# Gated attention in front of a soft mixture of experts and a tanh block: heads scored apart in 64x64 tiles, blocks of 64 tokens, one VectorE product a level

## The reference

```python
# q, k, v, f_logit: batch 4, heads 8, tokens 768, head_dim 48
f = 1.0 / (1.0 + np.exp(-f_logit))
state = zeros(B, H, D, D)
for t in range(S):
    state = f[:, :, t, :, None] * state + einsum('bhd,bhe->bhde', k[:, :, t], v[:, :, t])
    y[:, :, t] = einsum('bhd,bhde->bhe', q[:, :, t], state)
x = y as (3072 tokens, 384)
x = soft mixture of experts (x; phi 384x32, w1 8x384x1024, w2 8x1024x384)
out = (h - tanh(h)) @ w_out,  h = x @ w_in            # 384 -> 2048 -> 384
```

## Time and profile before

| what | value |
|---|---|
| time, median of 3 runs | 676.52 us (674.4 to 677.11) |
| span of the profiled execution, its own time | 674.4 us |
| PE busy | 581.7 us, 86%, 4505 instructions |
| DVE busy | 542.1 us, 80%, 970 |
| ACT busy | 214.4 us, 32%, 462 |
| POOL busy | 231.9 us, 34%, 294 |
| DMA | 55.39 MB, mean 82 GB/s |

### The profile page before, as it was taken

One profiled execution on the slowest core, in us unless ns is written; L12 is line 12 of the kernel. 1 busy time (PEld: TensorE's weight loads), 2 busy tenths in 40 slices (PEclk: granted clock), 3 DMA queues, 4 the chain that ended last, 5 costly groups with the idle time before them and its releaser, 6 DMA issues.

```text
span 674.4 us, 14283 instructions
## 1 busy us (share of the span) xinstructions
PE 581.7 (86%) x4505; PEld 504.7 (75%) x4505; DVE 542.1 (80%) x970; ACT 214.4 (32%) x462; POOL 231.9 (34%) x294
## 2 busy tenths in 40 slices
PE   4888878888888878888878888679999999999997
PEld 3767767677767767677765733269999999999997
DVE  4999999999999999999994642497777777777773
ACT  1233332334333332334323550312323223232322
POOL 3566565665666565665652000560000000000000
PEclk9899999999999999999999798879999999999999
DMA  5324433335253260533600689600100001010101
GB/s 102 69 44 91 127 70 111 70 60 156 41 139 70 52 163 17 146 76 63 205 1 1 201 287 394 242 0 1 48 0 16 31 0 47 0 47 0 47 1 47
DMA packets 118405, 55.39 MB, mean 82 GB/s; under 512 B 101616, under 2 KB 114928, under 8 KB 118000
## 3 DMA queue, kind: packets, MB, share of 16 engines
q1 hardware_dynamic: 118384, 55.11, 29.8%
HBM read 50.38 MB, written 4.72 MB: 82 GB/s over the span
## 4 chain that ended last, share of the span: by engine, by line
PE 53%; issue 26%; DVE 12%; POOL 3%; DMA 3%; ACT 1%; DVEq 1%; POOLq 1%; SPq 1%; ACTq 0%
PE level_ps L692 5%; PE level_ps L693 5%; PE y_ps L692 5%; PE level_ps L694 5%; PE y_ps L694 5%; PE y_ps L693 5%; PE turn_ps L469 4%; PE y_ps L493 4%; PE turn_ps L467 4%; POOL kd L394 3%; PE turn_ps L673 3%; DVE seg L855 3%; DMA w_second<-in_moe_w 2%; DVE state L938 2%; DVE scores L888 2%
## 5 line engine op out<-in xcount | busy, mean ns | idle before, releaser
L394 POOL TENSOR_TENSOR kd<-kd,seg 112x192 f32<-112x192 f32 x192 | 128.3, 677 | 105.2 <-PE turn_ps L467 54.8
L878 DVE TENSOR_TENSOR qd<-qd,seg 112x384 f32<-112x384 f32 x192 | 115.1, 600 | 2.5 <-PE level_ps L467 1.1
L467 PE MATMUL level_ps<-qd,kd 112*128 112x128 f32 x576 | 90.7, 294 | 28.1 <-DVE qd L878 25.0
L814 ACT ACTIVATE tanh_h<-turn_ps 128x512 f32<-128x512 f32 x96 | 57.4, 599 | 160.3 <-PE turn_ps L673 148.5
L467 PEld LDWEIGHTS level_ps<-qd,kd 112*128 112x128 f32 x576 | 73.2, 193 | 43.5 <-issue 29.9
L467 PE MATMUL turn_ps<-qd,kd 112*128 112x128 f32 x576 | 82.5, 288 | 23.6 <-DVE qd L878 22.2
L1069 DVE TENSOR_TENSOR g<-turn_ps,tanh_h 128x512 f32<-128x512 f32 x96 | 66.4, 692 | 40.6 <-ACT tanh_h L814 40.4
L467 PEld LDWEIGHTS turn_ps<-qd,kd 112*128 112x128 f32 x576 | 72.5, 194 | 31.8 <-issue 18.0
L692 PE MATMUL level_ps<-w_out_hi,g_hi 128*128 128x384 f32 x192 | 66.2, 345 | 6.6 <-DVE g_lo L1074 6.6
L1074 DVE TENSOR_TENSOR g_lo<-g,g_hi 128x512 fp32r<-128x512 f32 x96 | 68.8, 716 | 3.3
L733 ACT ACTIVATE scores<-turn_ps 16x96 f32<-16x96 f32 (+1 forms) x160 | 46.5, 291 | 68.9 <-DVE scores L888 54.4
(11 more groups left out here) (133 smaller groups left out, 909.1 us busy)
## 6 DMA issues: line engine op xcount, KB each, us to landing
w_sb<-in_moe_w SPq DMA_DIRECT2D x8, 1536.0 KB, 7.2
w_first<-in_moe_w SPq DMA_DIRECT2D x4, 1536.0 KB, 7.1
raw<-in_f_logit SPq DMA_DIRECT2D x32, 144.0 KB, 2.5
raw<-in_k SPq DMA_DIRECT2D x32, 144.0 KB, 3.0
raw<-in_q SPq DMA_DIRECT2D x32, 144.0 KB, 3.1
vt<-in_v SPq DMA_DIRECT2D x32, 144.0 KB, 2.8
w_second<-in_moe_w SPq DMA_DIRECT2D x3, 1536.0 KB, 10.5
out_rows_dram<-out_rows SPq DMA_DIRECT2D x24, 192.0 KB, 1.9
```

What stands on the lines that cost most here:

```text
L394: pool.tensor_tensor(kg, kg, halves(w, lv, g)[:, :, 1].unsqueeze(2).to_broadcast([R, nb, h]), ALU.mult).then_inc(k_ready, 1)
L467: mm = pe.matmul(bank[:, o], kd[w][0:R, t0:t0 + CH], mov[:, :, :, 1, :], start=True, stop=True)
L814: act.activation(tanh_h[ft % 2][:, :], h_banks[ft % 4], ACT.Tanh).then_inc(tanh_done, 1)
L878: dve.tensor_tensor(qs, qs, tot, ALU.mult).then_inc(q_ready, 1)
```

## The change

**Blocks of 64.** The levels stop at blocks of 64 tokens: six scored levels instead of seven, over all six chunks at once and not in two groups. The state is now made for 11 of 12 blocks (`block_states`) and carried over them (`carry`, 10 steps).

**Heads apart.** `level` scores each head of each block of 64 alone: 48 rows of keys, 64 columns of weights, 32 moving queries, at row offset 0 or 64 and column offset 0 or 64 of the array; 24 matmuls a level. The zeroed copy of the queries is gone: `qk[w]` holds queries and keys of a unit side by side.

**One product a level.** `move` multiplies the queries of second halves and the keys of first halves in one VectorE instruction of 768 elements a partition. GpSimd's `keys` are gone. The gates' totals are made a unit ahead (`products`, in `totals`).

**Merging and the diagonal.** VectorE merges levels 1 to 5, one instruction each for all chunks; ScalarE copies level 6 and writes the diagonal by 12 small scaled copies of an identity (`eye`). GpSimd keeps `multiply`, and makes masks of 5 levels and 192 columns, in two halves of partitions, at the start, behind its first `multiply`.

**Units pipelined.** On TensorE the transposes, block states, scores-times-values and states of unit n-1 and the loads' transposes of unit n+1 stand between the levels of unit n. SP waits for each of the three raw tensors apart. There is no loop over units any more: the code is written out.

The core of the diff:

```diff
-    HALF = CH // 2
-    LEVELS = 8
-    NEAR = 5
+    BK = 64
+    NB = S // BK
+    HALF = BK // 2
+    LEVELS = 6
+    NEAR = LEVELS - 1
+    LC = NC * HALF
...
-    kd = [place(f"kd{i}", [P, S]) for i in range(2)]
-    scores = [place(f"scores{i}", [P, NC * 2, CH]) for i in range(2)]
+    qk = [place(f"qk{i}", [P, 2, S]) for i in range(2)]
+    totals = [place(f"totals{i}", [P, S]) for i in range(2)]
+    scores = [place(f"scores{i}", [P, 2, NC, BK]) for i in range(2)]
+    state = place("state", [P, NB, D])
...
+            def unit(n, w):
+                if n < UNITS - 2:
+                    sp.wait_ge(turned, gates_set(n + 1))
+                    load_rows(n + 2, 0)
+                if 0 < n < UNITS - 1:
+                    sp.wait_ge(v_used, n)
+                    load_values(n + 1, 1 - w)
+                if n < UNITS - 2:
+                    sp.wait_ge(turned, gates_set(n + 1) + 1)
+                    sp.wait_ge(pairs_done, n + 2)
+                    load_rows(n + 2, 1)
+                    sp.wait_ge(turned, gates_set(n + 1) + 2)
+                    load_rows(n + 2, 2)
...
-                for lv in levels:
-                    if lv > 1:
-                        pool.wait_ge(seg_ready, n * (LEVELS - 1) + (lv - 1))
-                    for g in range(2):
-                        cols = slice(g * GT, (g + 1) * GT)
-                        pool.wait_ge(level_done, n * STEPS + (2 * (lv - 1) + g + 1))
-                        if lv > 1:
-                            pool.wait_ge(k_ready, n * STEPS + (2 * (lv - 2) + g + 1))
-                        if lv == 1 and g == 0:
-                            pool.wait_ge(dots_done, n + 1)
-                        kg = kd[w][0:R, cols].rearrange("r (n two h) -> r n two h", two=2, h=h)[:, :, 0, :]
-                        pool.tensor_tensor(kg, kg, halves(w, lv, g)[:, :, 1].unsqueeze(2).to_broadcast([R, nb, h]),
-                                           ALU.mult).then_inc(k_ready, 1)
+            for lv in range(1, LEVELS):
+                h = 1 << (lv - 1)
+                nb = HALF // h
+                for i in range(2):
+                    pool.wait_ge(consts_made, made)
+                    m = masks[BK * i:BK * (i + 1), lv - 1, :].rearrange("p (c n h) -> p c n h", c=NC, h=h)
+                    pool.affine_select(out=m, in_=m, compare_op=ALU.is_ge, fill=0.0, base=0,
+                                       pattern=[[0, NC], [-2 * h, nb], [0, h]],
+                                       channel_multiplier=1).then_inc(consts_made, 1)
+                    pool.wait_ge(consts_made, made + 1)
+                    pool.affine_select(out=m, in_=m, compare_op=ALU.is_ge, fill=0.0, base=h - 1,
+                                       pattern=[[0, NC], [2 * h, nb], [0, h]],
+                                       channel_multiplier=-1).then_inc(consts_made, 1)
+                    made += 2
+            pool.wait_ge(consts_made, made)
+            for n in range(1, UNITS):
+                pool.wait_ge(dots_done, n)
+                multiply(n)
...
-                    bank = level_banks[(2 * lv + g) % 4]
-                    for c in range(GC):
-                        t0 = (GC * g + c) * CH
-                        o = slice(c * P, (c + 1) * P)
-                        if lv < LEVELS - 1:
-                            mov = qd[w][0:R, :, t0:t0 + CH].rearrange("p a (n two h) -> p a n two h", two=2, h=h)
-                            mm = pe.matmul(bank[:, o], kd[w][0:R, t0:t0 + CH], mov[:, :, :, 1, :], start=True, stop=True)
-                        else:
-                            mm = pe.matmul(bank[0:HALF, o], kd[w][0:R, t0:t0 + HALF],
+            def level(n, w, lv, first):
+                h = 1 << (lv - 1)
+                if lv == 1:
+                    pe.wait_ge(turn_read, gates_set(n) + 2)
+                else:
+                    pe.wait_ge(moved, n * LEVELS + (lv - 1))
+                if lv > 2:
+                    pe.wait_ge(merged_near, n * NEAR + (lv - 2))
+                elif not first:
+                    if lv == 1:
+                        pe.wait_ge(merged_near, n * NEAR)
+                    else:
+                        pe.wait_ge(merged_far, n)
+                for c in range(NC):
+                    for b in range(2):
+                        t0 = c * CH + b * BK
+                        for a in range(2):
+                            r = slice(HP * a, HP * a + D)
+                            mov = qk[w][r, 0, t0:t0 + BK].rearrange("p (n two h) -> p n two h", two=2, h=h)
+                            mm = pe.matmul(level_bank(lv)[BK * b:BK * (b + 1), a * 512 + c * HALF:a * 512 + (c + 1) * HALF],
+                                           qk[w][r, 1, t0:t0 + BK], mov[:, :, 1, :], start=True, stop=True)
+                mm.then_inc(scored, 1)
...
+            def turn_keys(n, w):
+                pe.wait_ge(moved, n * LEVELS + LEVELS)
+                pe.wait_ge(turn_read, k_tok_set(n) - 1)
+                for c in range(NC):
+                    mm = pe.transpose(turn_ps[:, c * P:c * P + R], qk[w][0:R, 1, c * CH:(c + 1) * CH], ident[0:R, 0:R])
...
+            def block_states(n, w):
+                pe.wait_ge(turn_read, k_tok_set(n))
+                pe.wait_ge(v_loaded[w], n // 2 * 32 + 32)
+                for c in range(NC):
+                    for b in range(2):
+                        if 2 * c + b < NB - 1:
+                            for a in range(2):
+                                mm = pe.matmul(turn_ps[HP * a:HP * a + D, b * 512 + c * D:b * 512 + (c + 1) * D],
+                                               k_tok[BK * b:BK * (b + 1), c, HP * a:HP * a + D],
+                                               vt[w][BK * b:BK * (b + 1), a, c, :], start=True, stop=True)
+                mm.then_inc(turned, 1)
...
+            def across(n, w):
+                pe.wait_ge(state_step, n * STEPS + STEPS)
+                pe.wait_ge(v_used, n + 1)
+                for t in range(1, NB):
+                    c, b = t // 2, t % 2
+                    for a in range(2):
+                        r = slice(HP * a, HP * a + D)
+                        mm = pe.matmul(y_at(c, b, a), state[r, t - 1, :], qk[w][r, 0, t * BK:(t + 1) * BK],
+                                       start=False, stop=True, skip_group_check=True)
...
+            def unit(n, w, first, last):
+                level(n, w, 1, first)
+                if not first:
+                    turn_keys(n - 1, 1 - w)
+                level(n, w, 2, first)
+                if not first:
+                    block_states(n - 1, 1 - w)
+                level(n, w, 3, first)
+                if not last:
+                    turn(n + 1, 0)
+                if not first:
+                    within(n - 1, 1 - w, range(0, NC // 2))
+                level(n, w, 4, first)
+                if not first:
+                    within(n - 1, 1 - w, range(NC // 2, NC))
+                if not last:
+                    turn(n + 1, 1)
+                level(n, w, 5, first)
+                if not first:
+                    across(n - 1, 1 - w)
+                if not last:
+                    turn(n + 1, 2)
+                level(n, w, 6, first)
...
+            def diagonal(n, w):
+                act.wait_ge(dots_done, n + 1)
+                for a in range(2):
+                    for c in range(NC):
+                        x = act.activation(scores[w][:, a, c, :], eye[:, :], ACT.Copy, scale=dots[:, a, c:c + 1])
...
+            def unit(n, w, first, last):
+                if not first:
+                    finish_keys(n - 1)
+                    finish_states(n - 1)
+                if not last:
+                    act.wait_ge(moved, n * LEVELS + 1)
+                    take(n + 1, 0, 1 - w)
+                    take(n + 1, 1, 1 - w)
+                    diagonal(n + 1, 1 - w)
+                if not first:
+                    take_y(n - 1)
+                far(n, w)
...
-                qs = qg.rearrange("r a (n two h) -> r a n two h", two=2, h=h)[:, :, :, 1, :]
-                tot = halves(w, lv, g)[:, :, 0].unsqueeze(1).unsqueeze(3).to_broadcast([R, 2, nb, h])
-                dve.tensor_tensor(qs, qs, tot, ALU.mult).then_inc(q_ready, 1)
+            def move(n, w, lv):
+                h = 1 << (lv - 1)
+                dve.wait_ge(scored, n * LEVELS + lv)
+                if lv > 1:
+                    dve.wait_ge(totals_made, n * LEVELS + (lv - 1))
+                x = part(qk[w], h, [[2 * h, S // (2 * h)], [S - h, 2], [1, h]])
+                tile, off = total(w, lv)
+                t = part(tile, off, [[2, S // (2 * h)], [1, 2], [0, h]])
+                dve.tensor_tensor(x, x, t, ALU.mult).then_inc(moved, 1)
+            def merge(n, w, lv):
+                if lv > 1:
+                    dve.wait_ge(merged_near, n * NEAR + (lv - 1))
+                h = 1 << (lv - 1)
```

(34 more changed lines are left out.)

507 lines of the change are left out of this document (201 added, 306 removed).

## The result

The changed kernel takes 653.65 us (median of 6 runs, 646.08 to 661.73) where the kernel before takes 674.56 (6 runs, 671.31 to 677.11): ratio 0.9672, 95% interval 0.9618 to 0.9725. It is faster by 21 us; 56 were forecast. The profiled execution, 646.08 us, is the fastest of the six.

What follows compares the result with a forecast made beforehand. VectorE, busy 20.61 of 21.69 us a unit, was taken as the bound. 26.6 + 15.2 + 16.6 + 13 x 17.13 + 25.3 = 306.4, about 3 for slow clock, 308.4 unchanged: 618, stated as 620; range 596 to 668.

Steps and rivals of the forecast that it cites:

- The list of 15.3 us a unit: VectorE's work in a unit, added up from moves, merges, first queries, totals, diagonal and carries: 15.3 us against 20.6.
- The start: Before unit 0, VectorE waits for GpSimd's masks, so the first move comes at 26.6 us.
- The rest: The code behind attention that the change leaves alone: 308.4 us, taken as unchanged.
- the path of a unit: Chain through TensorE's levels and VectorE's moves, which wait for each other: 17.13 us a unit, against 21.69.
- The ring through q: From level 6 to level 3: q's buffer freed, loaded, multiplied, diagonal summed, level-2 move: 7.31 us.
- level instructions at 0.015: Cheaper price for TensorE's small level instructions, 0.026 being assumed; q's load would still hold a unit at 16.5 us.
- the sum's last but one: TensorE at its lower clock at the start only: about 3 us added to 306.4.
- The clock's rival: TensorE's clock falls to 1.2 GHz in the units: 21.8 us a unit, end 689; chance 0.13.
- Dearer tiles: TensorE's small level tiles cost 0.036 us an instruction: level 2.0, unit 18.8, end 646; chance 0.17.
- weights that wait: Each TensorE level matmul waits for its own weights, 0.058 us: unit 24.5, end 738; chance 0.05.
- Short runs: VectorE's move takes 1.75 us at levels h = 1 and 2: 18.1 a unit, 636; at all six, 674; chance 0.08.
- The sentence that short runs cost nothing: Runs of one element cost VectorE's move nothing extra, from a product at 0.56 against 0.55; move priced at 0.96 us.

Runs made afterwards that it cites:

- fill_more_masks_spread: Changed kernel with 16 unread 128x128 matmuls a unit, masks built for 32 columns and copied, w1 loads split in parts over two units: 610.40 us, ratio 0.9057.
- fill: Changed kernel with 13 unread 128x128 matmuls a unit put ahead of TensorE's waits: 631.36 us, ratio 0.933.
- split1: Changed kernel with the level-1 move alone done as two products of 384 elements: 660.59 us, ratio 0.9825.
- qbuf: Changed kernel with a second buffer for the q rows of odd units, loaded behind f: 657.31 us, ratio 0.9751.
- fill_masks: Changed kernel with 13 unread 128x128 matmuls a unit and masks built for 32 columns and copied to the rest: 623.51 us, ratio 0.9257.
- before_flat: Kernel before the change with only its loop over units written out: 671.61 us, ratio 0.9968.

## Why the prediction was right in direction and wrong in size

**Right: what bounded before, and how far VectorE falls.** The list of 15.3 us a unit came out at 14.8 to 15.0, though the level-1 move took 0.62 more than its term; moves 0.957 for 0.96 at five of six levels. The start: 27.7 for 26.6. The rest: 306.5 for 308.4.

**Right in its links, lucky in its sizes: the path of a unit, at the full clock.** In `fill_more_masks_spread` TensorE's levels start as follows:

```profile
223.88 0.90 PE L420 MATMUL level_ps<-qk 48*64 48x32 f32 x48
...
226.97 0.90 PE L420 MATMUL level_ps<-qk 48*64 48x32 f32 x48 [0.34 <-DVE qk L847]
...
229.05 0.90 PE L420 MATMUL level_ps<-qk 48*64 48x32 f32 x48
...
231.83 0.90 PE L420 MATMUL level_ps<-qk 48*64 48x32 f32 x48
...
236.27 0.90 PE L420 MATMUL level_ps<-qk 48*64 48x32 f32 x48
...
237.75 0.90 PE L420 MATMUL level_ps<-qk 48*64 48x32 f32 x48
```

2 to 3: 3.09 (forecast 3.26), 3 to 4: 2.08 (2.65), 4 to 5: 2.78 (2.65), 5 to 6: 4.44 (4.52), 6 to 1: 1.48 (1.40), and 2.63 are left of 16.50 for 1 to 2 (2.65). Two errors cancel in the last: a level costs 0.90 and not 1.51, the level-1 move 1.60 and not 0.96. 3 to 4 shows the cheaper level alone (0.57 less); 4 to 5 is TensorE's own list, transposes and a filler included, with no wait for VectorE. The ring through q closes the unit as described (6 to 3: 7.20, forecast 7.31; VectorE waits 0.60 us for the pairs). For level instructions at 0.015 the prediction named 16.5 us a unit; they took 0.0136, and the fourteen units 16.80 on average.

**Wrong: the clock.** The step that failed is the sum's last but one, "At the start TensorE runs at its lower level ... That adds about 3", with the sentence in the rival that "The new units keep it busy nearly all the time, which speaks against a fall". The clock was given 0.13 as a rival and no cost in the forecast beyond the start. It fell to a mean of 0.67 over 60 to 300 us.

Term by term, measured against forecast: the first move 1.1 us later; unit 0 16.30 for 15.2, 1.1 more; the fourteen units behind it 266.24 for 239.3 (16.6 and 13 x 17.13), 26.9 more; from the last level-1 move to TensorE's next stage 27.5 for 25.3, 2.2 more. Less the 3 us that were allowed, these are the 28.2 us by which that stage started late (337.71, forecast 309.5). The rest of the miss of 34 is that the median lies 9.5 above the profiled span, where 2.1 above the profiled time was allowed for, less 1.9 in the part behind attention.

That the 26.9 are the clock's is shown by the runs that change it. At 1.00 the fourteen units take 16.80 us each in `fill_more_masks_spread` and not 19.02, 31 us less, with 16 fillers more in each. `fill` raises the clock from 0.67 to 0.91 and saves 22 us, fillers of the small shape leave it at 0.68 and the kernel at 743.66, and six wide fillers lie between none and 13 in clock and time. With the clock held, and 9 us added back for the long masks, the time is 619, where the forecast was 620. That it is as near as 1 us is luck: the tiles were priced too dear, the level-1 move too cheap, and that kernel's loads are divided too. What in the small tiles lets the clock fall stays open.

**The clock's rival was mis-sized.** It priced a unit wholly at 1.2 GHz at 21.8 and the kernel at 689, slower than before. Units at 0.50 took 19.6 to 20.6, because a level of small tiles costs 1.51 there and not a quarter more than that. That is under the 20.8 from which it would have decided, so the sign held.

**The other rivals.** Dearer tiles (0.036) and weights that wait (0.058) are out: 0.0136 at full clock, 0.0266, (1.51 - 0.26)/47, at half. Short runs do slow a move, at level 1 (1.58 for 0.96) and not at level 2; at this kernel's clock the 0.6 us a unit cost nothing that `split1` could win back. The sentence that short runs cost nothing, read off a product with one run of one element after another, did not hold for a run that alternates between two places element by element.

## What to carry to other kernels

A change from wide to small tiles must be priced twice, at both levels of TensorE's clock, and the first price is only good if rows of the same kind of work show the full one; TensorE busy 26.51 of 26.51 us was no protection. When an engine's share falls and the gain stays out, read PEclk by unit before the waits: here two real savings (`qbuf`, `split1`) measured nothing, since another engine was the bound at the lower clock, and at the higher the ring (`split1`) or, in part, a collision with GpSimd (`qbuf`). And where TensorE shows gaps marked "issue" behind large loads, try those loads in parts: with 16 fillers that gave 13 us of 624, with 13 nothing.

## What the runs showed of the hardware that was not expected

- Tiles of 48 rows x 64 columns with 32 moving columns ran at 0.0136 us an instruction at the full clock and 0.0266 at the half one. The 48 weight loads of a level at the full clock took 0.79 us together (`fill_masks`). The Trainium skill ("TensorE: Matmul & The Clock Gate", section "LDWEIGHTS") gives a load of 64 columns 53 ns; the loads here don't bear that out.
- Fillers of the levels' own shape left the clock at 0.68 over 60 to 300 us, 128x128 ones brought it to 0.91.
- Before its first change PEclk says 1.00 whatever the clock is: `qbuf`'s unit from 44.79 to 64.58 reads 1.00 with six transposes at 1.53 us.
- 1.5 MB loads at 400 GB/s are followed by stops of TensorE of up to 2.3 us, 3.1 where eight came together, in the written-out code with small tiles; in `before_flat` by none of 0.5 us.
- GpSimd's select goes by runs: over 64 partitions 1.65 us for 192 runs and 0.43 for 12, so 6.8 ns a run; over 128 partitions it was 6.4 (0.66 for 64, 0.30 for 8). Half the partitions cost the same.
